# Query halves in the two column groups: one attention result and one folding per head

## The reference

```python
def _attn_ref(q, k, v, centroids):            # q, k, v: 2 x 8 x 768 x 64; centroids: 8 x 16 x 64
    q_assign = argmax over 16 centroids of normalised q . normalised c      # one cluster per query
    k_assign = the same for the keys
    mask = q_assign[:, :, :, None] == k_assign[:, :, None, :]
    scores = where(mask, (q @ k^T) / 8, -1e9)
    attn = exp(scores - max); attn = attn / (sum(attn) + 1e-9)
    return attn @ v

def reference(...):
    x = attention output, heads side by side      # 2 x 768 x 512
    u = x + real(fft over tokens and channels of x)
    x = u + relu(layernorm(u) @ w_ch1) @ w_ch2
    h = relu(x @ w_in); gate = sigmoid(conv of 3 tokens over h)
    return (h * gate) @ w_out
```

## Time and profile before

| what | value |
|---|---|
| median of 3 runs | 701.66 us (701.42 to 702.7) |
| the profiled execution | 703.32 us, span 701.5 us from first to last instruction |
| mean granted TensorE clock | 0.993 of full speed |
| busy share of the span | PE 98%, PEld 79%, DVE 48%, ACT 40%, POOL 35% |
| attention heads | about 28 to 264 us |
| share of the chain that ended last | PE 93%, DVE 5%, ACT 1%, issue 1% |

### The profile page before, as it was taken

The page is one execution under the profiler, slowest core; times in us unless marked ns, Lnnn a source line. Parts: engine busy times, 40 slices in busy tenths (PEclk is TensorE's granted clock), DMA queues, the critical chain, the costliest instruction groups (busy, mean ns, idle before and its releaser), DMA issues.

```text
span 701.5 us, 9821 instructions
## 1 busy us (share of the span) xinstructions
PE 689.7 (98%) x3714; PEld 555.8 (79%) x3714; DVE 337.9 (48%) x614; ACT 278.1 (40%) x538; POOL 243.4 (35%) x264
## 2 busy tenths in 40 slices
PE   8899999999999999999999999999999999999998
PEld 7676766767777779888888888888888899988876
DVE  4786776767766648843113211131111489933410
ACT  4676666666666632211112111121111377743411
POOL 5645869567597053488500000000150070000000
PEclk7999999999999999999999999999999999999999
DMA  5453444434443020133200000010040520000011
GB/s 174 135 149 82 131 113 117 116 79 108 142 145 88 1 69 31 47 112 112 61 0 1 0 1 1 0 61 1 10 171 0 175 67 1 0 31 31 30 46 45
DMA packets 25918, 47.04 MB, mean 67 GB/s; under 512 B 3728, under 2 KB 10768, under 8 KB 25616
## 3 DMA queue, kind: packets, MB, share of 16 engines
q1 hardware_dynamic: 23392, 38.08, 19.0%
q0 software_dynamic: 2336, 7.95, 3.5%
q10 hardware_dynamic: 144, 0.39, 0.2%
HBM read 35.98 MB, written 3.15 MB: 56 GB/s over the span
## 4 chain that ended last, share of the span: by engine, by line
PE 93%; DVE 5%; ACT 1%; issue 1%; POOL 0%; DVEq 0%; POOLq 0%
PE ps L1577 19%; PE ps L1543 19%; PE ps L1340 10%; PE ps L1625 9%; PE ps L1639 9%; PE ps L1325 8%; PE ps L1314 6%; PE ps L1315 5%; PE ps L1420 2%; PE ps L1349 1%; PE ps L1269 1%; PE ps L1390 1%; PE ps L1475 1%; PE ps L1286 1%; DVE gate L1208 1%
## 5 line engine op out<-in xcount | busy, mean ns | idle before, releaser
L1147 DVE SCALAR_TENSOR_TENSOR hid_l<-ps,hid_h 128x512 fp32r<-128x512 f32 x48 | 33.2, 692 | 197.4 <-ACT hid_h L802 197.4
L908 DVE TENSOR_REDUCE row_min<-ps 128x1 f32<-128x768 f32 x96 | 91.7, 955 | 67.6 <-PE ps L1315 67.6
L802 ACT ACTIVATE hid_h<-ps 128x512 fp32r<-128x512 f32 x48 | 28.7, 599 | 223.6 <-PE ps L1543 223.6
L694 ACT ACTIVATE prob<-ps,row_min 128x768 f32<-128x768 f32 x96 | 86.4, 900 | 19.3 <-DVE row_min L908 15.2
L1325 PE MATMUL ps<-cst,prob 128*128 128x128 f32 x576 | 79.0, 272 | 0.7 <-DVE pt L916 0.6
L1314 PE MATMUL ps<-k,q 80*128 80x384 f32 x192 | 75.5, 393 | 1.1 <-ACT prob L694 0.8
L1340 PE MATMUL ps<-pt,v_n 128*64 128x384 f32 x384 | 75.8, 503 | 0.5 <-DVE x L990 0.5
L1577 PE MATMUL ps<-w_h,hid_h 128*128 128x512 f32 x192 | 76.2, 397 | 0.0
L1577 PE MATMUL ps<-w_h,hid_l 128*128 128x512 f32 x192 | 75.5, 393 | 0.0
L1577 PE MATMUL ps<-w_l,hid_h 128*128 128x512 f32 x192 | 74.7, 389 | 0.0
L1325 PEld LDWEIGHTS ps<-cst,prob 128*128 128x128 f32 x576 | 68.8, 141 | 5.2 <-issue 1.9
(11 more groups left out here) (176 smaller groups left out, 1397.0 us busy)
## 6 DMA issues: line engine op xcount, KB each, us to landing
w_raw<-in_moe_w_ch SPq DMA_DIRECT2D x24, 256.0 KB, 2.5
raw_d<-in_q SPq DMA_DIRECT2D x8, 384.0 KB, 3.4
v_n<-in_v SPq DMA_DIRECT2D x16, 192.0 KB, 2.5
out<-out_s SPq DMA_DIRECT2D x12, 256.0 KB, 2.0
raw_qk<-in_k SPq DMA_DIRECT2D x15, 192.0 KB, 3.2
raw_qk<-in_q SPq DMA_DIRECT2D x15, 192.0 KB, 3.3
q<-q SPq DMA_DIRECT2D x15, 192.0 KB, 2.8
k<-k SPq DMA_DIRECT2D x15, 192.0 KB, 3.2
```

Of the source, the lines that this page charges most:

```text
L694: nc.scalar.activation(prob[t % 2][:, :, :].rearrange("p (h j) c -> p h (j c)", h=2), ps[:, 2 * (t % 2):2 * (t % 2) + 2, 0:HALF], ACT.Exp, ...
L908: nc.vector.tensor_reduce(row_min[:, col:col + 1], ps[:, 2 * (t % 2):2 * (t % 2) + 2, 0:HALF], axis=AX.XY, op=ALU.min).then_inc(min_ready, 1)
```

## The change

The two column groups hold the two halves of the queries instead of the even and odd key tiles. A key tile's values are loaded for both groups, group a multiplies them with `pt[a]`, and the sum over all six key tiles of both halves ends in one bank. There is one `store_o`, one `fold_o` of three transposes and one `store_x` per head. The number of value matmuls stays twelve per head. They stand in three blocks of four, of which the last is done in the next head. `store_x` is now a product with the inverse denominators that takes 384 numbers a row, and the two products on GpSimd in `fold_block` are gone. The waits are renumbered, the mask and dot work is put at other places on ScalarE and VectorE, and `last_head` is rewritten.

```diff
+VALUES_AT = ((0, (0, 1)), (2, (2, 3)), (4, (4, 5)))
...
             def load_v(i, s):
                 n = 2 * i + s
                 if n >= V_BUFS:
-                    sp.wait_ge(o_ready, AHEAD + 2 * (n - V_BUFS) + 2)
+                    sp.wait_ge(o_ready, AHEAD + n - V_BUFS + 1)
...
-                pool.wait_ge(rden_done, 2 * (step + 2) + 2)
-                pool.wait_ge(x_stored, AHEAD + 2 * (step + 2) + 2)
-                for i in (2 * j, 2 * j + 1):
-                    own = x[:, b, :, BLOCKS[i] * D:(BLOCKS[i] + 1) * D]
-                    by_row = rden[:, 2 * i + b, :, :].rearrange("p a r -> p (a r)")
-                    nc.gpsimd.tensor_tensor(own, own, by_row.unsqueeze(2).broadcast_to([P, NT, D]),
-                                            ALU.mult).then_inc(x_scaled, 1)
-                pool.wait_ge(x_scaled, 2 * fold_order(b, j) + 2)
+                pool.wait_ge(x_stored, AHEAD + step + 3)
...
             def head(n, s):                       # ScalarE
-                step(n, s, 4)
-                step(n, s, 5)
-                store_o(n, 0)
...
+                exponent(n, s, 5)
+                store_left(n, 4)
+                exponent(n + 1, 1 - s, 0)
+                if n:
+                    store_o(n - 1)
+                store_left(n, 5)
+                step(n + 1, 1 - s, 0)
...
-            def store_x(n, s, a, i):
-                dve.wait_ge(fold_ready, AHEAD + 2 * n + a + 1)
+            def store_x(n):
+                i, s = n // 2, n % 2
+                dve.wait_ge(fold_ready, AHEAD + n + 1)
+                dve.wait_ge(rden_done, 2 * n + 2)
                 at = BLOCKS[i] * D
-                nc.vector.tensor_reduce(x[:, s, R * a:R * a + R, at:at + D],
-                                        ps[:, o_bank(n, a), 0:HALF].rearrange("p (r e d) -> p r d e", r=R, e=2),
-                                        axis=AX.X, op=ALU.add).then_inc(x_stored, 1)
+                nc.vector.tensor_tensor(x[:, s, :, at:at + D].rearrange("p (a r) d -> p a r d", a=2),
+                                        ps[:, O_BANK, 0:HALF].rearrange("p (r a d) -> p a r d", r=R, a=2),
+                                        rden[:, s, :, :].unsqueeze(3).broadcast_to([P, 2, R, D]),
+                                        ALU.mult).then_inc(x_stored, 1)
...
             def last_head(i, s):                  # VectorE
...
                 z_low_part(0, Z_ORDER[0][0])
                 invert(n, 1)
-                store_x(n, s, 0, i)
+                store_x(n - 1)
                 z_low_part(0, Z_ORDER[0][1])
-                store_x(n, s, 1, i)
+                store_x(n)
...
+            def values(n, tiles):                 # TensorE
+                if tiles[0] == 0:
                     for stored in (left_stored, right_stored):
-                        pe.wait_ge(stored, 6 * n + 3 * a + 3)
+                        pe.wait_ge(stored, 6 * n + 6)
                     pe.wait_ge(v_loaded[n % V_BUFS], 16 * (n // V_BUFS + 1))
+                    if n:
+                        pe.wait_ge(x_stored, AHEAD + n)
+                for j in tiles:
+                    for a in range(2):
+                        last = nc.tensor.matmul(ps[a * D:(a + 1) * D, O_BANK, 0:HALF], v_n[n % V_BUFS][:, j, :],
+                                                pt[n % 2][a][:, j, :], start=j == 0, stop=j == NT - 1)
...
                 step(n, s, 4)
-                values(n, s, 0, 0)
+                if n:
+                    values(n - 1, VALUES_AT[2][1])
                 step(n, s, 5)
-                values(n, s, 0, 1)
-                if n % 2 and u < UNITS_M:
-                    turn_mask(u)
-                if n % 2 == 0 and u < UNITS_M:
-                    dots(u)
-                step(nxt, 1 - s, 0)
-                fold_o(n, 0)
+                if n:
+                    fold_o(n - 1)
+                step(nxt, 1 - s, 0)
+                if n % 2 == 0 and u < UNITS_M:
+                    dots(u)
+                values(n, VALUES_AT[0][1])
+                step(nxt, 1 - s, 1)
                 if n % 2 == 0 and u < UNITS_M:
                     turn_dots(u)
-                step(nxt, 1 - s, 1)
-                values(n, s, 1, 0)
+                if n % 2 and u < UNITS_M:
+                    turn_mask(u)
                 step(nxt, 1 - s, 2)
-                values(n, s, 1, 1)
+                values(n, VALUES_AT[1][1])
                 step(nxt, 1 - s, 3)
-                fold_o(n, 1)
...
             def last_head(n, s):                  # TensorE
                 turn(n, 4, 0)
-                values(n, s, 0, 0)
                 turn(n, 4, 1)
+                values(n - 1, VALUES_AT[2][1])
                 transform_tokens(0, Z_ORDER[0][0])
+                fold_o(n - 1)
                 turn(n, 5, 0)
                 turn(n, 5, 1)
-                values(n, s, 0, 1)
                 transform_tokens(0, Z_ORDER[0][1])
-                fold_o(n, 0)
-                values(n, s, 1, 0)
-                values(n, s, 1, 1)
+                values(n, tuple(range(NT)))
                 transform_tokens(0, Z_ORDER[0][2])
-                fold_o(n, 1)
+                fold_o(n)
```

More of the change, by code:

```diff
@@ L120, in build @@
         den = sb(att, "den", [2, R])
-        rden = sb(att, "rden", [NH, 2, R])
+        rden = sb(att, "rden", [2, 2, R])
         dot_max = sb(att, "dot_max", [4 * NT])
@@ L309, in z_count @@
             return ZS * b + Z_ORDER[b].index(m) + 1
-        def o_bank(n, a):
-            return 7 if n == NH - 1 and a else 6
+        O_BANK = 6
         ZS = 2 * KC + 1
@@ L702, in store_left @@
                 act.wait_ge(turn_ready, 2 * g + 1)
-                if t % R == 0 and n >= 2:
-                    act.wait_ge(o_ready, AHEAD + 2 * (n - 2) + a + 1)
+                if t == 0 and n >= 2:
+                    act.wait_ge(o_ready, AHEAD + n - 1)
                 nc.scalar.activation(
@@ L724, in head @@
             def head(n, s):
-                step(n, s, 4)
-                step(n, s, 5)
-                store_o(n, 0)
[L729 to L736, removed]
+                u = n // 2 + 2
+                exponent(n, s, 5)
[6 more added lines that the diff above has]
+                if n % 2 == 0 and u < UNITS_M:
+                    store_dots(u)
+                step(n + 1, 1 - s, 1)
+                if n % 2 and u < UNITS_M:
+                    store_mask(u)
+                exponent(n + 1, 1 - s, 3)
+                store_left(n + 1, 2)
                 step(n + 1, 1 - s, 3)
@@ L746, in last_head @@
             def last_head(n, s):
-                step(n, s, 4)
+                exponent(n, s, 5)
+                store_left(n, 4)
+                store_o(n - 1)
                 z_high_part(0, Z_ORDER[0][0])
-                step(n, s, 5, more=False)
-                store_o(n, 0)
+                store_left(n, 5)
                 z_high_part(0, Z_ORDER[0][1])
-                store_o(n, 1)
+                store_o(n)
             act.wait_ge(q_scaled, 1)
@@ L1012, in head @@
                 if masking:
-                    masks(u)
+                    first_hit(u)
                 step(n, s, 4)
@@ L1022, in head @@
                 store_right(m, 0)
-                store_x(n, s, 0, i)
+                if masking:
+                    masks(u)
+                minimum(m, 1 - s, 3)
+                store_right(m, 1)
                 if dotting:
                     largest_dot(u)
-                minimum(m, 1 - s, 3)
-                if dotting:
-                    hits(u)
-                store_right(m, 1)
-                if dotting:
-                    weigh_hits(u)
                 minimum(m, 1 - s, 4)
@@ L1034, in head @@
                 if dotting:
-                    first_hit(u)
+                    hits(u)
                 step(m, 1 - s, 3)
-                store_x(n, s, 1, i)
+                if dotting:
+                    weigh_hits(u)
             def last_head(i, s):
                 n = 2 * i + s
-                step(n, s, 4, more=False)
+                store_right(n, 4)
                 denominator(n, s, 0)
@@ L1327, in turn, with fold_o @@
                 last.then_inc(turn_ready, 1)
[L1329 to L1332 removed]
+            def values(n, tiles):
+                if tiles[0] == 0:
                     for stored in (left_stored, right_stored):
[L1334 removed]
+                        pe.wait_ge(stored, 6 * n + 6)
                     pe.wait_ge(v_loaded[n % V_BUFS], 16 * (n // V_BUFS + 1))
[L1336 to L1342 removed]
+                    if n:
[4 more added lines that the diff above has]
+                                                pt[n % 2][a][:, j, :], start=j == 0, stop=j == NT - 1)
+                if tiles[-1] == NT - 1:
                     last.then_inc(o_ready, 1)
[L1345 to L1347 removed]
+            def fold_o(n):
+                pe.wait_ge(o_stored, n + 1)
                 for r in range(R):
[L1349 to L1350 removed]
```

(1 more changed line is left out.)

41 lines of the change are left out of this document (15 added, 26 removed).

## The result

Median after 705.1 us (20 runs), before 702.69 (20 runs); ratio 1.0034, 95% interval 1.002 to 1.0048. A second set, timed again beside the kernel before, gave 1.0043 (1.0027 to 1.0058). The forecast was 697.2, that is 4.5 us less than the 701.66 it was counted from; measured are 2.4 us more. The profiled execution took 703.59, span 701.7.

A forecast was written before the change was run, and what follows sets the result against it. TensorE, busy 98% of the span, was taken as the bound. -10.9 + 2.2 + 0.5 + 0.4 + 0.3 + 0.15 + 0.45 + 2.4 = -4.5 us, from median 701.66 to 697.2; range 693.8 to 700.0.

The forecast's parts named there:

- Prices: TensorE in attention: bare step 1.38 us, block of four 1.64, folding 0.32; two heads in about 28.7 us.
- Right copy at direct pairs: VectorE's copy late where two steps follow directly, 18 places: 0.12 us each, 2.2 us in all.
- The first rival: Channel tables are in time, so no wait before the first channel transform: -6.9 us, 694.8; chance 0.14.
- the second: VectorE late at more places or by more: 2.7 to 4.5 us added, 699.9 to 701.7; chance 0.14.
- the third: At direct pairs of steps the right copy falls a whole VectorE piece behind: 7.7 us more, 704.9; chance 0.05.
- the fifth: Value matmul pairs stop overlapping, each 0.65 us instead of 0.325: 62 us more, 759; chance 0.02.
- (d): SyncE's value load waits about 4.3 us longer; q and k copies queued behind are needed much later: nothing booked.
- Term (c): The mask turn stands alone on TensorE, 0.32 us for 0.28, six times: 0.3 us with rounding.
- (g): End of attention: TensorE waits for GpSimd's channel tables before its first channel transform, 2.4 us, bounds 0 and 3.
- the fourth rival: TensorE's stand of 2.4 us drops its clock to 1.2 GHz, 5.2 us lost: 702.4, no change; chance 0.05.
- the 10.9 removed: TensorE work dropped in attention: 17 value blocks' fixed parts, 5.8 us, and 16 foldings, 5.1 us.
- the small waits: Late copies, waits for stores and the lone mask turn on TensorE, channel tables apart: 4.0 us booked.

The follow-up runs named there:

- the control: Kernel before with only the odd heads' mask work moved to where the change has it: ratio 1.004; with the making of the masks left in place, 1.0009.
- early masks: Changed kernel with the odd heads' mask turn, store and making back where they were before the change: ratio 0.9951 to the kernel before.
- all three edits: Changed kernel with odd heads' masks back early, dot rows loaded behind the next head's mask rows, channel tables loaded before folding head 14's x: 0.9889, later 0.9905.
- early tables: Changed kernel with both channel table loads issued ahead of the folding of head 14's x: ratio 0.9994 to the kernel before.
- late dot rows only: Changed kernel with only the 768 KB of q and k rows for dot products loaded behind the next head's mask rows: ratio 1.0072 to the kernel before.
- early masks and tables: Changed kernel with the mask work back early and channel tables loaded before folding head 14's x, dot rows left in place: 0.9932, later 0.9912.

## Why the prediction was wrong, step by step

**Prices: right.** Block of four 1.64, a bare step 1.38, two heads 28.63 without waits for 28.7 forecast.

**Right copy at direct pairs: right in the place looked at.** Turn to block after such a pair, in the changed kernel:

```profile
98.50 0.85 PEld L1325 LDWEIGHTS ps<-cst,prob 128*128 128x128 f32 x6
99.52 0.20 PEld L1339 LDWEIGHTS ps<-pt,v_n 128*64 128x64 f32 x4 [0.17 <-issue]
```

1.02 for the 0.92 of the earlier trace rows: 0.10 a place, 0.12 booked. The first rival (tables in time) did not happen, nor the second, the third or the fifth.

**(d) The value load and what is queued behind it, "so nothing": wrong, and this is the step that failed.** It set the q and k copies against a head "more than 10 us later". It left out the mask rows, which wait for a store that the change itself had moved behind two steps, and the cascade: SyncE's queue holds the mask rows, then the load that GpSimd waits for before it splits the next q and k. It also never asked what the spare of each first score was (how much earlier its rows are there than TensorE wants them): 9.1 us of work behind the mask turn against rows that need 5.5 to 8. The moved turn took 3.1 us of that (9.1 to 6.0, as in the control), the block and the folding that left the stretch 1.3 (6.0 to 4.7). Term (c) priced the moved turn by TensorE's own time alone, 0.3 us. Measured: 1.0 + 0.8 + 0.8 + 3.3 = 5.9 us for 0 booked.

**(g) Tables: right.** GpSimd's first sum 252.67, table issued 258.92, landed 4.9 later; first channel transform at 263.91, a stand of 2.17 (2.4 forecast), 11.24 from the sum (11.5). The landing answers to the earlier trace rows: 4.9 for 5.2. The estimate of 3.2 us that was worked out from the Trainium skill (DMA: Bandwidth & Descriptors, Anatomy of one DMA) would have left a stand of 0.4; the measurement decides against it, where a load of 645 KB stands right ahead.

**Clock: the fourth rival's mechanism came, beside the rest and smaller.** It was given 5.2 us from the start-up stretch. It costs 1.4 to 1.5 a time: from the first channel transform of the first batch to the third of the second (L1455 both) it is 20.51 us where the clock fell and 19.10 where it did not, behind a stand of 2.17 in both:

```profile
258.51 0.19 PEld L1455 LDWEIGHTS ps<-ch_h,z_h 128*128 128x128 f32 x1 [2.17 <-DVE z_l L1005]
...
277.61 0.19 PEld L1455 LDWEIGHTS ps<-ch_h,z_h 128*128 128x128 f32 x1 [0.69 <-DVE z_l L1090]
```

(early masks, no fall); the changed kernel has 263.91 and 284.42. The Trainium skill (TensorE: Matmul & The Clock Gate, HAM oscillation) describes a fall at waits for a DMA; the traces agree that it can happen (0.50 from 204 to 206 us, above), and not at each.

**The sum.** -4.5 + 5.9 (rows) + 1.5 + 1.4 (clock) - 0.2 (tables) = +4.1; measured +2.4 in the median. The traces show where the other 1.7 went. The first scores of head 1 load at 26 to 29 us, by chance of the run, so take the stretch from there to the first load of `w_h`, in the kernel before, the changed one and all three edits:

```profile
28.00 0.19 PEld L1314 LDWEIGHTS ps<-k,q 80*128 80x128 f32 x1 [1.02 <-issue]
293.60 0.19 PEld L1577 LDWEIGHTS ps<-w_h,hid_h 128*128 128x128 f32 x1
```

```profile
26.68 0.19 PEld L1314 LDWEIGHTS ps<-k,q 80*128 80x128 f32 x1 [1.03 <-issue]
294.19 0.19 PEld L1573 LDWEIGHTS ps<-w_h,hid_h 128*128 128x128 f32 x1
```

```profile
26.31 0.19 PEld L1315 LDWEIGHTS ps<-k,q 80*128 80x128 f32 x1 [1.03 <-issue]
283.69 0.19 PEld L1574 LDWEIGHTS ps<-w_h,hid_h 128*128 128x128 f32 x1
```

265.60, 267.51 and 257.38 us: the changed kernel loses 1.9, all three edits win 8.2. With no stand left, the 10.9 removed bring 8.2, so the small waits came to 2.7 where 4.0 were booked; which of them came short is not told apart. And behind a stand for rows the next heads are 0.10 shorter (14.56 for 14.66), 0.8 us in all: from the first scores of head 1 to those of head 15 the changed kernel takes 6.6 us more than all three, for 5.9 of stands and 1.5 of clock. +4.1 - 1.3 - 0.8 = 2.0, for 1.9 measured.

The chances were wrong in kind: a rival for "the loads of rows don't keep up" was missing, though each first score waits for them.

## What to carry to other kernels

When an engine that bounds a kernel is made faster, list what it waits for that is not made by another engine beside it but by a chain of loads, and read the spare of each from the trace before: time from the event that starts the chain to the use, less the chain. A moved producer comes off the same spare. If all spares are over the gain, book nothing; if not, move the start of the chain with the change.

## What the runs showed of the hardware

- Behind a stand of TensorE of 1.7 to 3.4 us the granted clock fell to 0.50 for 3 to 4 us in some executions and not in others. The shortest was 1.68 us (head 7, second set of the changed kernel); behind 3.17 us at head 13 it fell with early tables and stayed at 1.00 with late dot rows only; behind the tables' stand (2.17 to 2.37 us) it fell in three of seven profiles. Idle matmuls in two stands kept it at 1.00.
- Copies of 24 KB took 1.9 us from issue to landing and 6.6 with 768 KB issued 4 us ahead of them (early masks and tables); the same issues at the same distances took 4.7 in another execution (early masks), and the k copy beside them 9.1 and 6.7. So the landing of the same copy differed by about 2 us from one execution to another.
- In SyncE's queue a wait for one tile delays loads that have nothing to do with it: behind the late mask rows of head 5 the next weight load was issued at 82.4 us instead of 79.3, and TensorE waited 0.8 us at head 7; in the profile with the masks early that wait is gone.
